# Scores of an mLSTM kernel as four small matmuls a burst: even heads on the lower half of TensorE's rows, odd heads on the upper, instead of three heads in one block-diagonal matmul

## The reference

```python
for t in range(S):
    m_new = np.maximum(f_gate[:, :, t] + m, i_gate[:, :, t])
    f_stab = np.exp(f_gate[:, :, t] + m - m_new)
    i_stab = np.exp(i_gate[:, :, t] - m_new)
    m = m_new
    C = f_stab * C + i_stab * einsum('bhd,bhe->bhde', vt, kt)
    n = f_stab * n + i_stab * kt
    h_tilde = einsum('bhde,bhe->bhd', C, qt)
    denom = np.maximum(np.abs(nq), 1.0)          # nq = n . q
    y[:, :, t] = sigmoid(o_gate) * h_tilde / denom
...
h = np.maximum(xt @ w_tok1, 0.0) @ w_tok2        # xt: x with tokens last
u = x + h.transpose(0, 2, 1)
h2 = np.maximum(u @ w_ch1, 0.0) @ w_ch2
return u + h2
```

## Time and profile before

| | us |
|---|---|
| median of 3 runs | 456.21 (454.49 to 457.3) |
| the profiled execution's own time | 455.49 |
| span from its first to its last instruction | 453.8 |
| TensorE busy | 439.6 (97%), mean granted clock 0.995 |
| VectorE busy | 255.6 (56%) |
| ScalarE busy | 209.1 (46%) |
| GpSimd busy | 208.3 (46%) |

### The profile page before, as it was taken

One profiled execution on the slowest core, in us unless ns is written; L12 is line 12 of the kernel. 1 busy time (PEld: TensorE's weight loads), 2 busy tenths in 40 slices (PEclk: granted clock), 3 DMA queues, 4 the chain that ended last, 5 costly groups with the idle time before them and its releaser, 6 DMA issues.

```text
span 453.8 us, 9518 instructions
## 1 busy us (share of the span) xinstructions
PE 439.6 (97%) x3463; PEld 407.6 (90%) x3463; DVE 255.6 (56%) x592; ACT 209.1 (46%) x517; POOL 208.3 (46%) x293
## 2 busy tenths in 40 slices
PE   8899999999999999899999999999999999999996
PEld 3588988999999989799999998899999998999996
DVE  7689865777765356776674237666665326213122
ACT  3666459666554247654552137655652213211120
POOL 7535421789886333888861204798883000000000
PEclk9899999999999999999999999999999999999999
DMA  7557990443344415434454013534310010000101
GB/s 211 195 168 217 348 263 27 119 129 111 103 131 146 127 43 166 143 92 131 124 154 143 1 44 102 150 120 142 126 61 1 1 43 2 0 1 0 46 1 43
DMA packets 36616, 47.38 MB, mean 104 GB/s; under 512 B 3356, under 2 KB 29082, under 8 KB 36570
## 3 DMA queue, kind: packets, MB, share of 16 engines
q1 hardware_dynamic: 35674, 45.76, 33.4%
q10 hardware_dynamic: 896, 1.02, 0.6%
HBM read 42.73 MB, written 4.03 MB: 103 GB/s over the span
## 4 chain that ended last, share of the span: by engine, by line
PE 85%; DVE 5%; issue 4%; ACT 4%; DMA 1%; DVEq 0%; POOL 0%; POOLq 0%; ACTq 0%
PE pC L1165 32%; PE pA L1236 7%; PE pA L1237 7%; PE pA L1238 7%; PE pS L1077 6%; PE pA L1165 5%; PE pY L1134 4%; PE pA L1240 3%; PE pA L1241 3%; PE pC L1015 2%; PE pY L1113 2%; PE pN L1089 2%; DVE gb L856 1%; PE pA L1195 1%; DMA x<-o_gate_dram 1%
## 5 line engine op out<-in xcount | busy, mean ns | idle before, releaser
L988 DVE SCALAR_TENSOR_TENSOR h_lo<-pA,h_hi 128x384 fp32r<-128x384 f32 x96 | 53.5, 557 | 147.9 <-ACT h_hi L760 147.9
L760 ACT ACTIVATE h_hi<-pA 128x384 fp32r<-128x384 f32 x96 | 46.8, 488 | 138.7 <-PE pA L1241 138.6
L1165 PE MATMUL pC<-wc_hi,h_hi 128*128 128x320 f32 x288 | 94.1, 327 | 1.1 <-DVE wc_lo L846 1.0
L1165 PE MATMUL pC<-wc_lo,h_hi 128*128 128x320 f32 x288 | 88.7, 308 | 0.0
L1165 PE MATMUL pC<-wc_hi,h_lo 128*128 128x320 f32 x288 | 88.4, 307 | 0.0
L494 POOL TENSOR_TENSOR gb<-gb,pb 128x384 f32<-128x384 f32 (+1 forms) x54 | 49.1, 909 | 63.9 <-ACT pb L628 63.4
L1236 PE MATMUL pA<-uT_hi,wc_hi 128*128 128x384 f32 x192 | 65.2, 340 | 0.3 <-DVE wc_lo L846 0.3
L1237 PE MATMUL pA<-uT_lo,wc_hi 128*128 128x384 f32 x192 | 64.7, 337 | 0.0
L1238 PE MATMUL pA<-uT_hi,wc_lo 128*128 128x384 f32 x192 | 64.3, 335 | 0.0
L1165 PEld LDWEIGHTS pC<-wc_hi,h_hi 128*128 128x128 f32 x288 | 54.0, 188 | 2.3 <-DVE h_lo L988 1.3
L1165 PEld LDWEIGHTS pC<-wc_lo,h_hi 128*128 128x128 f32 x288 | 54.2, 188 | 0.1
(11 more groups left out here) (135 smaller groups left out, 881.6 us busy)
## 6 DMA issues: line engine op xcount, KB each, us to landing
gb<-g_dram SPq DMA_DIRECT2D x18, 512.0 KB, 3.9
kv<-kvN_dram SPq DMA_DIRECT2D x24, 324.0 KB, 4.0
kd<-kT_dram SPq DMA_DIRECT2D x24, 180.0 KB
qz<-qT_dram SPq DMA_DIRECT2D x72, 60.0 KB
out_dram<-u SPq DMA_DIRECT2D x24, 160.0 KB, 1.9
qd<-qT_dram SPq DMA_DIRECT2D x20, 180.0 KB, 2.6
gq<-g_dram SPq DMA_DIRECT2D x45, 60.0 KB
wc_raw<-w_ch_dram SPq DMA_DIRECT2D x6, 384.0 KB, 6.1
```

Of the source, the lines that this page charges most:

```text
L760: nc.scalar.activation(h2[0][:, slot % 2], pA[slot % 2][:, 0:HALF], ACT.Relu).then_inc(h2_hi, 1)
L988: nc.vector.scalar_tensor_tensor(h2[1][:, slot % 2], pA[slot % 2][:, 0:HALF], 0.0, h2[0][:, slot % 2].bitcast(F32), ALU.max, ALU.subtract) ...
L1165: ins = mm(dst, a[p], b[q], start=first and n == 0, stop=last and n == 2)
```

## The change

Keys and queries now lie in one tile `kq`, with heads 0, 2, 4, 6 on partitions 0 to 39 and heads 1, 3, 5, 7 on partitions 64 to 103, without zeros. Each head's scores are a matmul of their own: contraction over 40 rows, 128 columns. The eight heads of a chunk go in two **bursts** of four (`SCORED`), in the steps g = 0 and g = 1; the step g = 2 has none. Even heads' scores go to `pS`; odd heads' to `pC0` in batch 0 and to columns 128 to 511 of `pN` later, whose columns 0 to 122 still take the state. VectorE's product of a step becomes two instructions, one a bank. TensorE's wait before a burst is now for the product of the step before in batch 0 too, where it could be one step ahead. For later batches the state matmul of step m-1 is moved ahead of the burst of step m, and waits and counts are added that keep the bank `pN` to one of TensorE and VectorE. A chunk's keys and queries come with two DMAs instead of four; the memset and its semaphore are gone.

```diff
+SCORED = [(0, 1, 2, 3), (4, 5, 6, 7), ()]
+BURSTS = 2
...
-        kd = sb("kd", [ROWS, R, NG, L])
-        qz = sb("qz", [ROWS, R, NG, GH, L])
+        kq = sb("kq", [128, R, 2, H // 2, L])
...
+        def scores_place(ba, head):
+            pair, odd = divmod(head, 2)
+            if not odd:
+                return pS, pair * L
+            if ba == 0:
+                return pC[0], pair * L
+            return pN, L + pair % 3 * L
...
-                    sp.wait_ge(s_mm, NG * (n - R + 1))
+                    sp.wait_ge(s_mm, BURSTS * (n - R + 1))
...
-                sp.dma_start(kd[:, r], kT[ba, c]).then_inc(ready, 16)
-                for j in range(GH):
-                    rows_j = slice(j * D, (j + 1) * D)
-                    sp.dma_start(qz[rows_j, r, :, j, :], queries[rows_j, :, :]).then_inc(ready, 16)
+                for odd in range(2):
+                    sp.dma_start(kq[64 * odd:64 * odd + D, r], kq_pairs[ba, c, odd]).then_inc(ready, 16)
...
-            nc.vector.memset(qz[:, :, :, :, :], 0.0).then_inc(mem_ready, 1)
...
-                dve.wait_ge(s_mm, k + 1)
+                dve.wait_ge(s_mm, bursts(ba, c, g))
+                if ba > 0 and g >= BURSTS and c < NC - 1:
+                    dve.wait_ge(n_mm, NG * (NC - 1) * ba + m)
                 dve.wait_ge(e_exp, k + 1)
-                nc.vector.tensor_tensor(tile, scores_bank(ba, m)[:, 0:n * L].rearrange("p (h t) -> p h t", h=n), tile,
-                                        ALU.mult).then_inc(p_ready, 1)
+                for odd in range(2):
+                    heads = [h for h in range(GH * g, GH * g + n) if h % 2 == odd]
+                    tile = gb[:, c % Q, heads[0]:heads[-1] + 1:2, :]
+                    where, col = scores_place(ba, heads[0])
+                    sums = where[:, col:col + len(heads) * L].rearrange("p (h t) -> p h t", t=L)
+                    last = nc.vector.tensor_tensor(tile, sums, tile, ALU.mult)
+                last.then_inc(p_ready, 1)
...
-                held = 2 if ba == 0 else 1
-                if k >= held:
-                    pe.wait_ge(p_ready, k - held + 1)
-                mm(scores_bank(ba, m)[:, 0:n * L], kd[0:n * D, r, g, :],
-                   qz[0:n * D, r, g, 0:n, :].rearrange("p h t -> p (h t)"),
-                   start=True, stop=True).then_inc(s_mm, 1)
+                if k >= 1:
+                    pe.wait_ge(p_ready, k)
+                if ba > 0:
+                    pe.wait_ge(n_read, NG * (NC - 1) * ba + min(max(m - 1, 0), NG * (NC - 1)))
+                for head in SCORED[g]:
+                    pair, odd = divmod(head, 2)
+                    rows = slice(64 * odd, 64 * odd + D)
+                    last = mm(scores_of(ba, head), kq[rows, r, 0, pair, :], kq[rows, r, 1, pair, :],
+                              start=True, stop=True)
+                last.then_inc(s_mm, 1)
...
+                if ba > 0:
+                    pe.wait_ge(p_ready, STEPS * ba + m + 1)
                 mm(pN[0:n * D, 0:n * E1], kv[:, r, GH * g * D:(GH * g + n) * D],
...
             def attention(ba, m):
+                if ba > 0 and 1 <= m <= STEPS - NG:
+                    step_state(ba, m - 1)
                 if m < STEPS:
                     step_scores(ba, m)
...
-                if 1 <= m <= STEPS - NG:
+                if ba == 0 and 1 <= m <= STEPS - NG:
                     step_state(ba, m - 1)
```

More of the change, by code:

```diff
@@ L79, in step_in, with program @@
     return slot - BEHIND if b == 0 else slot + AHEAD
-def program(nc, qT, kT, kvN, i_gate, f_gate, o_gate, w_tok1, w_tok2, w_ch1, w_ch2, out):
+def program(nc, kq_pairs, qT, kvN, i_gate, f_gate, o_gate, w_tok1, w_tok2, w_ch1, w_ch2, out):
     ctx = ExitStack()
@@ L163, in program, with scores_of @@
         pN = bank("pN")
-        def scores_bank(ba, m):
-            return [pS, pC[0]][m % 2] if ba == 0 else pS
+        def scores_place(ba, head):
[5 more added lines that the diff above has]
+            return pN, L + pair % 3 * L
+        def scores_of(ba, head):
+            where, col = scores_place(ba, head)
+            return where[:, col:col + L]
         def turned_bank(s):
@@ L188, in program @@
         out_done = [sem(f"out_done{i}") for i in range(2)]
-        mem_ready = sem("mem_ready")
         ident_ready = sem("ident_ready")
@@ L303, in program, with bursts @@
         O_PARTS = ((0, NC - 2), (NC - 2, NC))
-        QK_DMAS = 4
+        def bursts(ba, c, g):
+            return BURSTS * (NC * ba + c) + min(g, BURSTS - 1) + 1
+        QK_DMAS = 2
         GQ_DMAS = 3
@@ L386, in _ @@
             load_values(0, 0)
-            sp.wait_ge(mem_ready, 1)
             load_scores(0, 0)
@@ L1070, in step_scores @@
                 k = STEPS * ba + m
-                n, r = HEADS[g], c % R
+                r = c % R
+                if not SCORED[g]:
+                    return
                 if g == 0:
                     pe.wait_ge(qk_in[r], 16 * QK_DMAS * (ba * (NC // R) + c // R + 1))
-                held = 2 if ba == 0 else 1
-                if k >= held:
-                    pe.wait_ge(p_ready, k - held + 1)
-                mm(scores_bank(ba, m)[:, 0:n * L], kd[0:n * D, r, g, :],
-                   qz[0:n * D, r, g, 0:n, :].rearrange("p h t -> p (h t)"),
-                   start=True, stop=True).then_inc(s_mm, 1)
+                if k >= 1:
[8 more added lines that the diff above has]
+                last.then_inc(s_mm, 1)
             def step_state(ba, m):
@@ L1279, in rows, with paired @@
         return np.ascontiguousarray(padded.reshape(B, NG, ROWS, NC, L).transpose(0, 3, 2, 1, 4))
+    def paired(a):
+        return a.reshape(B, H // 2, 2, NC, L, D).transpose(0, 3, 2, 5, 1, 4)
     def by_partition(w, k):
@@ L1289 @@
     arrays = {
-        "qT": rows(q), "kT": rows(k),
+        "kq_pairs": np.ascontiguousarray(np.stack([paired(k), paired(q)], axis=4)),
+        "qT": rows(q),
         "kvN": np.ascontiguousarray(np.concatenate([tokens(k).reshape(B, S, DM), values.reshape(B, S, H * E1)], axis=2)),
```

2 lines of the change are left out of this document (removed).

## The result

The kernel after takes **478.26 us** (median of 4 runs, 472.62 to 481.63), the one before 455.99 beside it (4 runs, 454.49 to 457.3). The ratio is 1.041, with a 95% interval of 1.0357 to 1.0462: slower by 4%, where 453.3 us had been forecast and 469 was the upper end of the range. The mean granted clock is another in each: 0.96 and 0.953 in the two shorter ones, 0.939 and 0.936 in the longer. By an estimate from these means, about 38 us of the shortest run passed at the half clock, and 58 us of the profiled one.

A forecast was written before the change was run, and what follows sets the result against it. TensorE, busy for 97% of the span, was taken as the bound; -2.9 - 0.7 + 0.8 - 0.4 + 0.3 = -2.9 us on 455.5 gave 452.6, forecast as a 453.3 us median. Own range 450 to 457, whole range 447 to 469.

The forecast's parts named there:

- The single bank: Batch 0: TensorE's wait for the product before each burst, 1.63 us against 1.66 between products, just covered, so nothing.
- SyncE: Loads: two DMAs a chunk fewer and slightly fewer bytes, which nothing waits for, so no change in time.
- -0.7 + 0.8 - 0.4: Batch 0, in us: bursts where TensorE leads, split products where VectorE leads, one burst replacing two steps' scores at the end.
- Batch 0 becomes a relay: Rival, batch 0: burst and product wait for each other in series, +6 us on the forecast, 459.3 us; chance 0.06.
- The memset: Start: removing its 1.98 us gains nothing, since it ended before a scan that sat idle 0.52 us for a DMA.
- Passes of a burst: Each burst: eight passes in five slots, 0.54 us, as matmuls start in order and only neighbours on different halves overlap.
- rival on loads: Bursts' weight loads: one by one, 469 us, chance 0.30; or unhidden by their own half's matmul, near 504, chance 0.06.
- Going in and out: Each burst: changing the array's division and back costs 0.25 us, ends 0.21 to 0.35; over 0.35 the prediction is wrong.
- The chunk before: Dense part of the kernel before: a chunk's scores cost 0.65 + 0.65 + 0.43 = 1.73 us.
- the 2.9 forecast: Batches 1 to 3: a chunk's bursts take 1.57 us against 1.73, so 18 chunks save 2.9 us.
- VectorE: Split products: 128 columns take about 0.2 us between starts; VectorE stays off the chain in batches 1 to 3.

The follow-up runs named there:

- e5: The kernel after, with SyncE waiting for batch 0's o gates before loading chunk 1's keys, queries and values: 474.34 us, ratio 1.0339.
- e7: The kernel before, with TensorE in batch 0 too waiting before a score matmul for the product of the step before: 456.51 us, ratio 1.0037.
- e11: e7 with each product split into two VectorE instructions, still with the old matmuls: 457.48 us, ratio 1.007.
- e10: e5 with bursts in batch 0 only and the old block-diagonal scores in batches 1 to 3: 469.72 us, ratio 1.0333.
- e2: The kernel after, with 30 unused matmuls filling TensorE's 6.6 us wait for the first exponentials: 475.64 us in the median, one run at 459.33.
- e1: The kernel after, with SyncE waiting for batch 0's o gates before the first four weight loads: 477.0 us, ratio 1.0394.
- e3: The kernel before, with the first four weight loads moved ahead of the first keys and queries in SyncE's queue: 459.4 us, ratio 1.010.
- e4: e1 with the heads of a burst in the order even, even, odd, odd: 480.8 us in the median.
- e9: Bursts in batches 1 to 3 only, with batch 0's scores, banks and loads as in the kernel before: 453.85 us, ratio 0.9983.
- e13: e11 with batch 0's score matmuls from step 3 on over half their columns: four runs of 456.09 to 459.81 us, six of 467.86 to 473.18.
- e8: e5 with three bursts a chunk, of 3, 3 and 2 heads, instead of two of 4: 482.18 us.
- e14: e5 with each burst of batch 0 issued twice: 468.82 us, ratio 1.0277.
- e6: e5 with three unused matmuls of 512 columns ahead of each burst of batch 0: 462.69 us, ratio 1.0184.
- e12: e6 with one filler matmul a burst instead of three: 485.49, 462.77, 473.67 and 464.78 us.

## Why the prediction was wrong

**The step that failed** is batch 0: "The single bank: TensorE now waits for the product before each burst … It is nothing here, but has no room", and with it "SyncE issues two DMAs a chunk fewer and moves slightly fewer bytes: nothing waits for that". Both were priced in waits at a fixed clock. The single bank's wait was there, 0.42 us at 28.83 and 1.04 in e5 at 35.70. Priced as a wait it comes to little: 1 to 2 us in e7, and 3 with the split products in e11 (the sum had +0.8 for the split). But a wait also leaves TensorE empty, and behind such waits the granted clock fell, for 31 us in e5 and 51 in the kernel after. No term of the sum held that: batch 0 was forecast at -0.7 + 0.8 - 0.4, and bursts in batch 0 alone measure 1.0333 (e10), 15 us. The wait alone isn't the whole cause either: with it, the block-diagonal scores kept the clock in six runs of seven (e7) and five of five (e11). The rival "Batch 0 becomes a relay" had the wait, at a chance of 0.06, and gave 459.3 us, near the run of e2 at full clock (459.33). Even it lacked the clock, the other 19 us of the result.

The profile before could have warned. Its own clock falls once, from 12.7 to 16.1 us, about this wait for ScalarE, and its mean is 0.995:

```profile
12.93 0.39 PE L1042 MATMUL pA<-above,eye 128*128 128x256 bf16 x1 [1.86 <-ACT gb L676]
```

Among its own runs beside the experiments, 52 of them, one took 464.91 us at a mean clock of 0.977. Beyond that point VectorE sets the pace, but TensorE has 23.58 of 24 us busy: with a bank in hand it could run ahead and stay full. The change took both: the bank, and a part of the work that had kept it full, since eight passes now go in four slots. The Trainium skill names this case (TensorE: Matmul & The Clock Gate, Part 1, "A second HAM failure mode: psum-queue depth-cycling"): small idle times between groups of matmuls, from cycling through banks, are enough to make the clock change. The trace agrees, with waits of 0.3 to 1.0 us ahead of the falls in the kernel after, e2 and e5; but here it doesn't swing to and fro, it stays low for 51 us, and in e7 and e11 such waits were not enough.

**SyncE.** A faster queue was taken for harmless. Its early loads run against ones that something waits for: the o gates came at 13.2 instead of 8.6 us. That was worth about 3 us: e5 with the gates at 9.8 us has a ratio of 1.0339 for 1.0394 in e1, and e3 has its last stage 3 us later with the gates at 10.8.

**The memset** "ended before the scan that follows it", and was nothing for VectorE, as said. It was something for SyncE, which no longer waits for `mem_ready` before the queries: `kq` is issued at 2.18 us, `kd` and `qz` stood at 3.37 to 9.3.

**Passes of a burst**: five slots forecast, four measured. The condition that the forecast set against it, matmuls that start in order, e4 refutes. The Trainium skill has the same condition (TensorE: Matmul & The Clock Gate, Part 3, The mechanism: "MATMULs are pc-monotone in start AND end"); here the measurement differs and decides, the first odd pass at 0.01 us behind the first even one with three even passes between them in the program. **Loads**: neither rival on loads came true. They lie under their own half's matmuls, and side by side, 0.01 us apart. The Trainium skill says so of different tiles (TensorEngine Tiling (Array Packing), Key Properties: "Different tiles can execute LdWeights and Matmul in parallel"), and the trace agrees. **Going in and out** was mis-sized: 0.25 was taken, 0.36 to 0.40 measured, over the bound of 0.35 above which the prediction called itself wrong. The two errors nearly cancel, 0.80 to 0.84 us a burst for 0.785; that the sum came near is luck. The chunk before stands, 1.73 us. So the gain is 0.09 us a chunk and not 0.16, 1.6 us over 18 chunks for the 2.9 forecast, of which the runs show 0.7 (e9, at most 1.5). Where the rest went is shown only in part: the stage beside batch 1 gains nothing (89.57 us in e9, 89.23 in e10), and single waits move a stage by more than is to be explained.

**VectorE**: a product of 128 columns takes 0.20 us from start to start, as forecast:

```profile
108.28 0.28 DVE L874 TENSOR_TENSOR gb<-pS,gb 128x128 f32<-128x128 f32 x1
108.48 0.41 DVE L874 TENSOR_TENSOR gb<-pN,gb 128x256 f32<-128x256 f32 x1
```

It stays off the path in batches 1 to 3, where TensorE waits 1.8 us for the products' low parts `pb` (L1162), 1.6 before.

What stays open: how much of the fall is due to gaps and how much to the bursts themselves, be it the half rows, the shorter work or the ends. Shown is that gaps can do it without tiles (e13, six runs of ten), and that all but one of the 32 runs of kernels with bursts in batch 0 and no wide filler had it (the kernel after, e1, e2, e4, e5, e8, e10, e14), though the gaps ahead of it in the kernel after were shorter than some that e7 came through. Bursts in batch 0 with a second pair of banks, so that TensorE could be a step ahead, were not run.

## What to carry to other kernels

Where the bound engine is TensorE, a change that makes its work shorter in a stretch led by another engine doesn't save that time; it empties TensorE, and the granted clock may fall for far longer than the gap. So read the clock per window first, and put the tiled form only where TensorE is dense (e9: no loss, and hardly a gain). Keeping a bank in hand where TensorE and VectorE hand work to and fro is the other thing to try; no run shows that it would have saved this change. And a queue that gets faster issues later loads sooner: look up whose load they then share the DMA engines with.

## What the runs showed of the hardware

- Two halves of 64 rows work as two streams, whatever the order in the program: starts 0.01 us apart with even, even, odd, odd as with pairs (e4). Loads too run side by side, 182 to 189 ns each (after).
- Changing from the whole array to halves and back costs 0.36 to 0.40 us a burst (after), spread over four places: before the first pass, between the first and the second, behind the last, and behind the first full matmul (0.09, 0.10, 0.10 and 0.11 us more than usual). A shorter burst pays as much, 0.41 (e8).
- The clock fell to 1.2 GHz after starts 0.6 to 1.4 us apart in an otherwise busy stream (after, e2, e5, e13), and held through starts up to 1.19 us apart in e7. Once low it stayed so for 31 to 61 us (14 in e14), although TensorE then showed 24.00 of 24 us busy (after); it came back as the second layer of batch 0 went on.
- The same program can hold or lose it: 462.77 to 485.49 us in e12, 456.09 to 473.18 in e13.
- Work added to the bound engine made a kernel faster (e6, 7 us less than the shorter runs of e5, with 33 more matmuls); work taken away made it slower in six runs of ten (e13, 11 us).
